# Attention unit loop of a fused attention and feed-forward kernel: v in two places and asked for two units ahead, raw weights one unit sooner, fewer products of zeros at the start

## The reference

```python
q_d = q.reshape(B, H, Sd, factor, D).mean(axis=3)      # k_d, v_d alike
out_up = np.repeat(sm_attn(q_d, k_d, v_d), factor, axis=2)
mask = np.abs(pos[:, None] - pos[None, :]) < factor
scores = np.where(mask, scale * np.matmul(q, k.transpose(0, 1, 3, 2)), -1000000000.0)
...
out_local = np.matmul(attn, v)
x = out_up + out_local            # then, with moe and moe2 weights (gate 1.0, 1.702):
h = x @ w_in;  g = h * (1.0 / (1.0 + np.exp(-gate * h)));  x = g @ w_out
```

## Time and profile before

| | us |
|---|---|
| median of 3 runs | 814.86 |
| lowest and highest | 814.63 and 815.61 |
| profiled execution, its own time | 815.39 |
| its span, first to last instruction | 813.6 |
| what lies around the span | 1.79 |

### The profile page before, as it was taken

One profiled execution on the slowest core, in us unless ns is written; L12 is line 12 of the kernel. 1 busy time (PEld: TensorE's weight loads), 2 busy tenths in 40 slices (PEclk: granted clock), 3 DMA queues, 4 the chain that ended last, 5 costly groups with the idle time before them and its releaser, 6 DMA issues.

```text
span 813.6 us, 15682 instructions
## 1 busy us (share of the span) xinstructions
PE 801.9 (99%) x5800; PEld 776.5 (95%) x5800; DVE 654.1 (80%) x944; ACT 538.8 (66%) x865; POOL 192.5 (24%) x199
## 2 busy tenths in 40 slices
PE   9999899999999999999999999999999999999998
PEld 5777699999999999999999999999999999999998
DVE  7999889999998767998768888899655688555466
ACT  5889776578745677655678555677455687455773
POOL 5789786720045420235300000000000000000000
PEclk9999999999999999999999999999999999999999
DMA  7887668776868797677887777878887778877873
GB/s 241 230 253 226 162 198 276 256 284 218 287 209 275 262 322 249 210 264 252 277 292 249 231 253 253 270 234 272 283 289 253 266 252 265 301 251 262 279 254 137
DMA packets 98331, 205.42 MB, mean 252 GB/s; under 512 B 8432, under 2 KB 56048, under 8 KB 98256
## 3 DMA queue, kind: packets, MB, share of 16 engines
q1 hardware_dynamic: 98256, 204.42, 76.5%
HBM read 160.87 MB, written 43.52 MB: 251 GB/s over the span
## 4 chain that ended last, share of the span: by engine, by line
PE 81%; POOL 8%; DVE 7%; issue 4%; ACT 0%; POOLq 0%; DVEq 0%; ACTq 0%
PE hid L330 42%; PE yp L356 36%; DVE gr L547 2%; POOL vpair L980 2%; POOL pband L974 2%; DVE wh L302 2%; POOL vavg L984 1%; PE yp L372 1%; DVE xs L257 1%; POOL G L1005 1%; POOL G L1004 1%; POOL G L1008 1%; PE pt L1183 0%; POOL G L1010 0%; POOL x L271 0%
## 5 line engine op out<-in xcount | busy, mean ns | idle before, releaser
L330 PE MATMUL hid<-xs,wh 128*128 128x384 f32 x2016 | 351.5, 334 | 1.3 <-DVE hw L516 0.8
L330 PEld LDWEIGHTS hid<-xs,wh 128*128 128x128 f32 x2016 | 349.4, 188 | 2.5 <-issue 2.0
L356 PE MATMUL yp<-gr,wh 128*128 128x384 f32 x1968 | 342.1, 334 | 0.0
L356 PEld LDWEIGHTS yp<-gr,wh 128*128 128x128 f32 x1968 | 341.2, 188 | 0.0
L293 ACT ACTIVATE wh<-wr 128x1024 fp32r<-128x1024 f32 (+1 forms) x164 | 164.6, 1003 | 151.4 <-PE hid L330 121.3
L547 DVE TENSOR_TENSOR gr<-G,gr 128x768 fp32r<-128x768 f32 x144 | 137.9, 964 | 52.6 <-ACT gr L428 52.6
L428 ACT ACTIVATE gr<-G 128x768 fp32r<-128x768 f32 x144 | 121.8, 846 | 66.8 <-PE yp L356 66.8
L302 DVE TENSOR_TENSOR wh<-wr,wh 128x1024 fp32r<-128x1024 f32 x76 | 89.9, 1182 | 15.4 <-ACT wh L293 15.1
L391 ACT ACTIVATE G<-G 128x1152 f32<-128x1152 f32 x48 | 55.7, 1161 | 1.1 <-DVE G L542 1.1
L511 DVE TENSOR_TENSOR hv<-p,hid 128x384 f32<-128x384 f32 x48 | 26.3, 548 | 29.2 <-PE hid L330 29.2
L537 DVE TENSOR_TENSOR G<-hv,hid 128x384 f32<-128x384 f32 x48 | 26.4, 550 | 29.1 <-PE hid L330 28.8
(11 more groups left out here) (101 smaller groups left out, 782.7 us busy)
## 6 DMA issues: line engine op xcount, KB each, us to landing
wh<-rests SPq DMA_DIRECT2D x72, 512.0 KB, 3.8
wr<-sums_out SPq DMA_DIRECT2D x48, 512.0 KB, 4.8
wr<-in_w_out SPq DMA_DIRECT2D x36, 512.0 KB, 5.4
rests<-wh SPq DMA_DIRECT2D x36, 512.0 KB, 3.4
wr<-sums_in SPq DMA_DIRECT2D x40, 384.0 KB, 4.0
wr<-in_w_in SPq DMA_DIRECT2D x40, 256.0 KB, 3.6
qk<-in_qkT SPq DMA_DIRECT2D x11, 576.0 KB, 7.1
G<-in_w_in SPq DMA_DIRECT2D x12, 512.0 KB, 5.5
```

The source lines that it names most:

```text
L330: last = eng.matmul(hid[:, at, 0:HALF], lhsT=wh[:, w % SLOTS, part, a % 4, cc * P:(cc + 1) * P], rhs=xs[:, rest, q, cc, :], start=start an ...
L356: last = eng.matmul(yp[:, at + m, 0:HALF], lhsT=wh[:, w % SLOTS, part, p % 4, m * P:(m + 1) * P], rhs=gr[:, p, rest, :], start=start and p ...
```

## The change

Five edits, all in the attention part.

1. `vn` becomes a list of two places: the old tile, and a part of the feed-forward tile `yt` that nothing else uses during the attention. Unit n uses place n mod 2, and there is one semaphore for each.
2. v is asked for two units ahead: at the start for units 0 and 1, and behind `v_half` of unit n for unit n+2. `load_vwin` of unit n+1 now stands ahead of that wait, and no longer behind it.
3. The raw weights of pair p are asked for in unit 2p-1, no longer in unit 2p (pair 0 stays in unit 0), with two semaphores.
4. `WARM` goes from 11 to 8, `IDLE` from (7, 6) to (4, 6).
5. SP's first weight loads for the feed-forward part, issued behind the last unit, also wait for the last `v_half`.

```diff
-        self.w0_in, self.w0_sum = sem("w0_in"), sem("w0_sum")
+        self.w0_in, self.w0_sum = [sem(f"w0_in{i}") for i in range(2)], sem("w0_sum")
...
-    WARM = 11
-
-    IDLE = (7, 6)
+    WARM = 8
+
+    IDLE = (4, 6)
...
-            vn = sb("vn", [HP, 2, FACTOR * 2 * D])[:]
+
+            vn = [sb("vn", [HP, 2, FACTOR * 2 * D])[:], ffn.yt[0:HP].rearrange("p a m n -> p (a m n)")[
+                :, 0:2 * FACTOR * 2 * D].rearrange("p (j n) -> p j n", j=2)]
...
             def load_vn(u):
-                eng.dma_start(vn, v[bass.ds(u.n, 1), :, :].rearrange(
-                    "a (p j r) d -> (a p) j (r d)", j=2, r=FACTOR)).then_inc(vn_in, DMA_INC)
+                eng.dma_start(vn[u.odd], v[bass.ds(u.n, 1), :, :].rearrange(
+                    "a (p j r) d -> (a p) j (r d)", j=2, r=FACTOR)).then_inc(vn_in[u.odd], DMA_INC)
...
                 load_vwin(u)
                 load_qk(u.after().after())
+                load_vn(u.after())
                 load_vwin(u.after())
...
-                if u.n + 1 < UNITS:
+                if u.n + 1 < UNITS and not first:
+                    eng.wait_ge(band_out, u.n)
+                    load_vwin(u.after())
+                if u.n + 2 < UNITS:
                     eng.wait_ge(v_half, u.n + 1)
-                    load_vn(u.after())
-                    if not first:
-                        eng.wait_ge(band_out, u.n)
-                        load_vwin(u.after())
-                if not u.odd:
+                    load_vn(u.after().after())
+                if first:
+                    ffn.first_raw(eng, 0)
+                elif u.odd and u.n + 1 < UNITS:
                     if u.half:
                         eng.wait_ge(ffn.w0_sum, 4 * u.half - 2)
-                    ffn.first_raw(eng, u.half)
+                    ffn.first_raw(eng, u.half + 1)
...
                 eng.wait_ge(band_out, UNITS)
+                eng.wait_ge(v_half, UNITS)
                 ffn.load_pair(eng, q)
...
-                eng.wait_ge(vn_in, DMA_INC * (u.n + 1))
+                eng.wait_ge(vn_in[u.odd], DMA_INC * (u.half + 1))
...
-                    eng.wait_ge(ffn.w0_in, DMA_INC * (p + 1))
+                    eng.wait_ge(ffn.w0_in[p % 2], DMA_INC * (p // 2 + 1))
```

More of the change, by code:

```diff
@@ L115, in first_raw @@
                              self.w_in[0][bass.ds(p, 1)].rearrange("a p n -> (a p) n")).then_inc(
-                                 self.w0_in, DMA_INC)
+                                 self.w0_in[p % 2], DMA_INC)
     def first_place(self, p, a):
@@ L856, in build @@
         vwin_in = [sem(f"vwin_in{i}") for i in range(2)]
-        vn_in = sem("vn_in")
+        vn_in = [sem(f"vn_in{i}") for i in range(2)]
         qk_in = [sem(f"qk_in{i}") for i in range(3)]
@@ L975, in body @@
                                   ALU.mult).then_inc(b_nrm, 1)
-                eng.wait_ge(vn_in, DMA_INC * (u.n + 1))
+                eng.wait_ge(vn_in[u.odd], DMA_INC * (u.half + 1))
                 if not first:
                     eng.wait_ge(v_sum, u.n)
-                rows = vn.rearrange("p j (r d) -> p r j d", r=FACTOR)
+                rows = vn[u.odd].rearrange("p j (r d) -> p r j d", r=FACTOR)
                 eng.tensor_tensor(vpair[:], rows[:, 0:2], rows[:, 2:4], ALU.add).then_inc(v_half, 1)
```

## The result

| | kernel before | changed kernel |
|---|---|---|
| 15 runs each: median | 814.86 us | 820.39 us |
| lowest and highest | 814.41 and 816.6 | 813.44 and 825.95 |
| changed to before | | 1.0045, interval 1.0026 to 1.0064 |
| profiled execution: time, span, clock | 815.39, 813.6, 1.000 | 824.0, 822.2, 0.994 |

The changed kernel is slower by 0.45%, outside the range of 810.3 to 814.3. Its runs spread over 12 us, and the longer ones have the lower granted clock: 1.0 at 813.44, 0.998 at 818.79, 0.994 at 824.0, 0.992 at 825.95. Ratios leave disturbed runs out, here the one of 825.95. The profiled execution of the changed kernel is 3.6 us above the median, so its stops and clock show more than the usual harm.

What follows compares the result with a forecast made beforehand. Attention was taken as bound by TensorE up to unit 8, then by GpSimd and VectorE. Gains 1.15 (v) + 1.12 (raw weights) + 0.39 (start) = 2.66 us gave 812.2 us at the median, range 810.3 to 814.3.

Steps and rivals of the forecast that it cites:

- What bounds the kernel: Attention: TensorE bounds up to unit 8, then GpSimd and VectorE; TensorE waits five times for `pband`, 5.1 us together.
- v, 1.15 us: Asking for v two units ahead removes GpSimd's waits of 0.21 and 1.22, counted as 0.21 plus 0.94.
- raw weights, 1.12 us: Asking one unit sooner removes GpSimd's waits of 0.43 and 0.69, both counted in full.
- 0.69 and 0.94: 0.69: GpSimd's raw-weight wait, counted in full; 0.94: TensorE's stall, counted for GpSimd's 1.22 wait for v.
- The 0.43: GpSimd's wait for raw weights ahead of TensorE's 0.81 stall, counted in full as gain.
- collision: GpSimd operation longer than its 0.73 when VectorE starts a split within 0.25 us; three together 2.99 too much; unit 14 reversed.
- The 0.21: GpSimd's wait for v, taken to lie ahead of TensorE's 0.57 stall and counted in full.
- Order on SP: SP's transfers: windows ahead of the `v_half` wait, one v moved to the start; cost nothing, cover a unit or more each.
- Rival 3: Transfers are late because the queue is full and come late again; only the start's 0.39 remains: 814.5 us, chance 0.04.
- Start, 0.39 us: Three warm-up products fewer: real work starts at about 4.80 instead of 5.19; gain 0.39 us, bounds 0 and 0.68.
- Rivals 1 and 2: 1: waits and collisions both go, 810.5 us, chance 0.15; 2: collisions take the waits' gain, 814.2, chance 0.23 with in-between cases.
- Rival 4: At the start TensorE stays at 1.2 GHz longer: 813.8 us, possibly 817.1; chance 0.08, of which 0.04 ends slower.

Runs made afterwards that it cites:

- experiment 3: Changed kernel with only the windows put back behind the wait for `v_half` and behind v: 814.29 us, 0.9979; with the start as before too, 0.9959 and 0.9988.

## Why the prediction was wrong

- **What bounds the kernel.** Right. With the waits for transfers gone and the queue as before (experiment 3), the `pband` waits fell from 5.1 to 2.46; 5.08 less the terms 1.15 and 1.12 makes 2.81.
- **v, 1.15 us, and raw weights, 1.12 us.** The sum is near, 2.62 gone against 2.27 forecast, but partly by luck. Stall by stall, before and with the order put back: 0.81 and 0.81, 0.55 and 0.55, 1.24 and 0.55, 0.94 and none, 1.54 and 0.55. So 0.69 and 0.94 came as forecast. The 0.43 was eaten by the collision behind it, now 2.30 instead of 1.83. The 0.21 could not count: GpSimd's wait ended at 73.62, behind the stall that it was put ahead of:

```profile
73.56 0.82 PE L1183 MATMUL pt<-ident,pband 128*70 128x128 f32 x6 [0.55 <-POOL pband L974]
```

And the 0.99 of the last stall, which was to stay, was not in the sum. The terms don't add up either: alone, v (windows behind) leaves 3.18 and the raw weights leave 3.16. In time the raw weights are worth 0.997 and 0.9982, 1.5 to 2.4 us, and v alone nothing (0.9998).

- **Order on SP: "Cost nothing; the cover is a unit or more for each".** This step failed. It asked of each transfer who waits for it, and found nobody near. It left out what waits for no transfer of data: TensorE's program, which is read by DMA as well. In the changed kernel landing went from 7.1 to 12.9 us, the stops at block borders from 0.40 to 6.63 us, and the clock cost up to 5.1 more. Even its own question had another answer: with landings near 13 us TensorE waited 0.72 for the windows. Rival 3 had the right object, a full queue, but took it for something that only limits the gain; it has to be asked what else the queue carries.
- **Start, 0.39 us.** First transposes at 11.73 instead of 11.96 in the changed kernel, 11.58 with the order put back: 0.23 and 0.38. But the old start gave 11.45 to 12.90 in the other profiles and the new one 13.05 in one: when the clock rose, between 3.7 and 10.0 us, mattered more than three products. In time: nothing that can be measured.
- **Rivals 1 and 2.** With the order put back the four collisions are all GpSimd's, 1.86 to 2.30 instead of 0.73, that of unit 14 too, and VectorE's splits are not held: neither rival, and for unit 14 not the forecast either.
- **Rival 4: "gaps of 1.54 us did not bring the clock down".** It looked only at the start, and took waits for `pband` as proof for all gaps. Stops of 1.32, 1.55, 1.96, 2.19, 2.21, 2.26, 2.33, 2.56 and 2.61 lie next to a fall, and so do two waits for data (1.82 for q and k, 3.67 for the windows); but stops of 1.19, 1.22, 1.46, 1.69, 1.81 and 2.01 and a wait of 2.31 do not. What tells them apart wasn't found.
- **The number.** The forecast of 812.2 is a gain of 0.33%. Without the full queue the changed kernel gained 0.48% (fewer window bytes) and 0.21% (order put back), one on each side of it. Slower had 0.05; the queue deserved far more, since in the kernel before the DMA engines were already busy to 78.3%.

What is shown: the harm needs both the lead and the order (as far as their intervals part), is absent with fewer bytes or the old order, and sits in TensorE's stops and the clock; and the stops are late program blocks: in every profile that has one it ends 1.30 to 1.76 us behind a 16 KB read, at a border between blocks.

What is argued: that the reads are late *because* data stands ahead of them. The landings fit, as they were long before the stops and not only behind them: in the changed kernel (above), and with v two ahead and the windows ahead of it, whose median of 7.4 us hides it. There q and k asked for between 14 and 34 us took 10.1 (`qk`) and 9.3 (`wt`), against 7.1 and 6.6 in the kernel before, and the stop at 34.64 follows. Those asked for at 84.7 took 11.3, ahead of the stop at 93.94. Between the stops they took 4.2 to 8.7. But the windows ahead alone had landings of 10.5 to 11.8 for what was asked for between 3.8 and 14 us, and no stop; the kernels with a second transfer of v and with q and k two ahead landed after 11.1 and 10.3 us and had one such stop each up to 105 us, and raw weights alone had one of 1.46 at 6.1. So landing alone does not foretell a stop. No run moved the program's reads alone. Raw weights sooner with the windows ahead, but v one unit ahead as before, was not tried either.

Against the kernel before, the raw weights alone are the best supported gain: 0.997 and 0.9982, both intervals below 1. With v in the old order as well it was 0.9959 the first time, but 0.9988 (0.9971 to 1.0004) the second, which is no clear gain; with the shorter start too, 0.9979, measured once. The intervals overlap, so these runs don't rank them; the simplest, one edit, gives what there is.

## What to carry to other kernels

Asking for data sooner is free only while the queue has room: where the DMA engines are busy to nearly 80% as here, compare the time from issue to landing before and after, and count the harm also for what waits for no data. When a stop "issue" lies within a group of products and comes at the same few counts of products in run after run, look for a read of the engine's own program that ends just ahead; here fewer bytes or the old order made such stops rarer. Where the profile names an engine that had long been done, look for a transfer that landed. And when an order is changed together with a lead, time them apart: each was harmless here, both together cost 0.3 to 0.5%.

## What the runs showed of the hardware

- TensorE stopped at the products 216, 338, 461 (460 in one run), 582, 705, 827, 950, 1073, 1196, 1318, 1440 and 1561, whatever line stands there: 0.33 to 2.61 us, each stop ending 1.30 to 1.76 us behind the end of a 16 KB read of program.
- Next to some of them the granted clock was 0.50 for 3.4 or 6.8 us; at half speed that is up to 1.7 or 3.4 us lost each, an estimate, about as much as the stop itself.
- A higher share of the DMA engines was not more bytes: from 24 to 32 us 212 GB/s at a share of 0.89, where the kernel before had 241 at 0.82.
- The Trainium skill (SBUF — State Buffer, section "SBUF: two separate sides") lets the engine that started first keep the port. With the order put back GpSimd's operation at 57.30 took 2.30 and those at 70.25, 82.77 and 95.30 1.86 to 1.87, though VectorE's splits started behind them (57.80, 70.58, 83.10, 95.62) and took their usual 1.22 and 0.95: the trace does not agree, as in the earlier trace rows.
